# Attention and token mixer: the last 64 queries of two heads share one score tile

## What is computed

```
q_rot, k_rot = rotate(q), rotate(k)                    # rotary embedding
scores = (q_rot @ k_rot.T) / sqrt(64)                  # 576 x 576 for each head
attn   = exp(scores - max(scores)); attn /= sum(attn) + 1e-9
x      = heads side by side of attn @ v                # [4, 576, 512]
h      = relu(x.T @ w_tok1) @ w_tok2                   # mixing over positions
u      = x + h.T
out    = u + relu(u @ w_ch1) @ w_ch2                   # mixing over channels
```

## Time and profile before

| | before |
|---|---|
| median of 3 runs (lowest to highest) | 741.0 us (741.0 to 745.12) |
| the profiled execution | 744.22 us, of which the span (first to last instruction) is 742.5 |
| TensorE matmul (PE) busy | 698.0 us, 94% of the span |
| VectorE (DVE) / ScalarE (ACT) / GpSimd (POOL) busy | 401.4 / 344.8 / 229.7 us |
| granted TensorE clock, mean | 0.995 |

### The profile page before, as it was taken

How to read it: one execution, slowest core, us unless ns; L and a number is a source line. 1 busy time by engine, 2 the same in 40 slices (tenths; PEclk the granted TensorE clock), 3 DMA queues, 4 the chain that set the end, 5 groups by cost and what they waited for, 6 DMA issues and landing times.

```text
span 742.5 us, 13143 instructions
## 1 busy us (share of the span) xinstructions
PE 698.0 (94%) x5104; PEld 657.6 (89%) x5104; DVE 401.4 (54%) x644; ACT 344.8 (46%) x743; POOL 229.7 (31%) x257
## 2 busy tenths in 40 slices
PE   2799999999999999988899999999999999999996
PEld 1688888898888888887799998999989999899996
DVE  6588998888888988887661213212232122221211
ACT  3488888888888888876340203102022021220110
POOL 3967777777777777222000000000000000000000
PEclk9999999999999999999899999999999999999999
DMA  8655666655666555760520001200012000000000
GB/s 225 151 143 147 153 159 147 152 149 145 156 141 149 148 147 124 180 233 17 187 72 1 29 1 36 72 1 29 1 36 71 0 28 0 12 25 1 29 1 35
DMA packets 58421, 65.56 MB, mean 88 GB/s; under 512 B 18432, under 2 KB 42112, under 8 KB 58368
## 3 DMA queue, kind: packets, MB, share of 16 engines
q1 hardware_dynamic: 58368, 64.84, 32.7%
HBM read 29.16 MB, written 9.44 MB: 52 GB/s over the span
## 4 chain that ended last, share of the span: by engine, by line
PE 50%; DVE 1%; ACT 1%; issue 0%; ACTq 0%
PE slot L903 14%; PE slot L904 14%; PE slot L902 14%; PE slot L943 4%; PE slot L936 1%; PE slot L990 1%; PE slot L166 1%; PE slot L169 1%; ACT x_hi L149 1%; PE slot L168 0%; DVE x_lo L154 0%; DVE x_hi L158 0%; ACTq L867 0%; DVE out_t L1111 0%; DVE out_t L1114 0%
## 5 line engine op out<-in xcount | busy, mean ns | idle before, releaser
L629 ACT ACTIVATE prob<-slot,neg_max 128x576 f32<-128x576 f32 x160 | 117.5, 737 | 41.4 <-DVE neg_max L719 41.4
L719 DVE TENSOR_REDUCE neg_max<-slot 128x1 f32<-128x576 f32 x160 | 115.2, 752 | 38.9 <-PE slot L503 38.0
L1036 ACT ACTIVATE h_hi<-slot 128x512 fp32r<-128x512 f32 (+1 forms) x48 | 31.3, 652 | 184.2 <-PE slot L904 184.2
L902 PE MATMUL slot<-ut_hi,w_ch_hi 128*128 128x320 f32 (+1 forms) x384 | 114.0, 297 | 0.0
L904 PE MATMUL slot<-ut_hi,w_ch_lo 128*128 128x320 f32 (+1 forms) x384 | 113.7, 296 | 0.0
L903 PE MATMUL slot<-ut_lo,w_ch_hi 128*128 128x320 f32 (+1 forms) x384 | 113.7, 296 | 0.0
L902 PE MATMUL slot<-h_hi,w_ch_hi 128*128 128x320 f32 (+1 forms) x384 | 113.7, 296 | 0.0
L903 PE MATMUL slot<-h_lo,w_ch_hi 128*128 128x320 f32 (+1 forms) x384 | 113.7, 296 | 0.0
L904 PE MATMUL slot<-h_hi,w_ch_lo 128*128 128x320 f32 (+1 forms) x384 | 113.7, 296 | 0.0
L1081 DVE SCALAR_TENSOR_TENSOR h_lo<-slot,h_hi 128x512 fp32r<-128x512 f32 (+1 forms) x56 | 41.5, 748 | 119.6 <-ACT h_hi L1036 112.9
L559 PE MATMUL slot<-ident,prob 128*128 128x128 f32 (+1 forms) x640 | 87.4, 276 | 1.8
(11 more groups left out here) (88 smaller groups left out, 1317.4 us busy)
## 6 DMA issues: line engine op xcount, KB each, us to landing
q_hi<-t_hi_q SPq DMA_DIRECT2D x32, 160.0 KB, 2.5
q_cross<-t_lo_q SPq DMA_DIRECT2D x32, 160.0 KB, 2.6
q_cross<-t_hi_q SPq DMA_DIRECT2D x32, 160.0 KB, 2.7
key<-t_hi_k SPq DMA_DIRECT2D x32, 160.0 KB, 2.8
key<-t_lo_k SPq DMA_DIRECT2D x32, 160.0 KB, 2.9
raw_qk<-in_q_dram SPq DMA_DIRECT2D x16, 256.0 KB, 2.7
raw_qk<-in_k_dram SPq DMA_DIRECT2D x16, 256.0 KB, 2.6
raw_v<-in_v_dram SPq DMA_DIRECT2D x16, 256.0 KB, 2.7
```

What stands on the lines that cost most here:

```text
L629: act.activation(prob[a][:, t, 0:S].rearrange("p (f n) -> p f n", f=2), slot[(a * NG + t) % 2][:, :, 0:HALF], ACT.Exp, bias=neg_max[a][:, ...
L719: dve.tensor_reduce(neg_max[a][:, t:t + 1], slot[(a * NG + t) % 2][:, :, 0:HALF], AX.XY, ALU.max, negate=True).then_inc(maxed[t], 1)
L902: pe.matmul(ps, lhs[0], rhs[0], start=first, stop=False)
L1036: act.activation(h2[0][:, 2 * i:2 * i + 2, 0:n], unit_slot(k)[:, :, 0:n], ACT.Relu).then_inc(hi_done, 1)
```

## The change

Heads are worked on in pairs, an even head and the odd one after it. The pair's last 64 queries share one tile: the raw q of the tail is laid block-diagonally (head 0's tail in partitions 0 to 63 and channel half 0, head 1's in partitions 64 to 127 and half 1, zeros elsewhere), so that column group 4 of the transposed q holds 64 queries of each head, and the tile's 128 rows are scored in three passes straight from `t_hi` and `t_lo` of q and k (six matmuls instead of four). The even head has five score tiles, the odd one four: nine for a pair. The same holds for `maximum`, `exponent`, the sums and the reciprocals (one for a pair).

The shared tile is transposed once, in two units of the even head: unit 5 (four 128×128 transposes) for the first 512 keys and unit 6 (one transpose) for the last 64. Their columns go to both ends of `pt_hi` and `pt_lo`, which become 640 wide: head 0's tail queries in columns 0 to 63, head 1's in 576 to 639, the main ones between. The odd head has units 0 to 4 alone. Each of units 5 and 6 is one instruction on ScalarE and one on VectorE.

```diff
-    UNIT_BANK = (3, 0, 1, 2, 3, 2)
+    TILES_PAIR = 2 * G + 1
+    UNIT_BANK = ({6: 2, 0: 3, 5: 2, 1: 0, 2: 1, 3: 2, 4: 3}, {0: 3, 1: 2, 2: 0, 3: 1, 4: 3})
+    UNITS = ((6, 0, 5, 1, 2, 3, 4), (0, 1, 2, 3, 4))
...
+                if t < G:
+                    cols = slice(t * P, (t + 1) * P)
+                    passes = ((q_hi[a][:, cols], key[a]), (q_cross[a][:, cols], key[a]))
+                else:
+                    pe.wait_ge(t_lo_done, 2 * p + 2)
+                    cols, i = slice(MAIN, W), p % 2
+                    passes = ((t_hi["q"][i][:, cols], t_hi["k"][i]), (t_hi["q"][i][:, cols], t_lo["k"][i]),
+                              (t_lo["q"][i][:, cols], t_hi["k"][i]))
...
-                    pe.wait_ge(pt_lo_done[1], m - 3)
-                    pe.wait_ge(pt_lo_done[2], m - 3)
+                    pe.wait_ge(pt_lo_done, units_until(m - 4, 2 if m % 2 == 0 else 3))
...
                 act.wait_ge(pt_ready, units_until(h, u))
+                if u == UNITS[a][0] and h > 0:
                     act.wait_ge(pv_ready, h)
...
+                elif u == 5:
+                    part, ps = tail_columns(pt_hi[:, 0:G, :]), ps.rearrange("p (j e n) -> p j e n", j=G, e=2)
                 else:
...
+                    part = tail_columns(pt_hi[0:TAIL, G:NG, :])
+                    ps = ps[0:TAIL, HALF:HALF + P].rearrange("p (j e n) -> p j e n", j=1, e=2)
+                act.activation(part, ps, ACT.Copy).then_inc(pt_hi_done, 1)
...
+                copy_o(odd - 2)
+                p_hi(even, 6)
+                exponent(odd, 2)
...
+                p_lo(even, 6)
+                maximum(odd, 2)
+                output(odd - 2)
```

More of the change, by code:

```diff
@@ L370, in step @@
                     assemble_k(0, buf)
-                late = isinstance(s, int) and s < 2
-                if ahead and not late:
+                if ahead and s >= 2:
                     sp.wait_ge(products, s * 2 + 10)
@@ L384, in step @@
                         assemble_k(1, buf)
-                if ahead and late:
+                if ahead and s < 2:
                     sp.wait_ge(products, s * 2 + 10)
                     load("qk"[a], p + 3)
[L389 to L395, removed]
+            for s in range(N):
+                step(s)
             for c in range(CT):
@@ L437, in normalise @@
                 if no(h):
                     return
[L439 to L445, removed]
-            for m in (2, 3):
-                rotate(pool, "qk"[m % 2], m)
@@ new lines, in values @@
+                a = h % 2
+                pe.wait_ge(v_split, h + 1)
+                for f in range(2):
+                    at = a * D + f * HALF
+                    for j in range(NG):
+                        if f == 0 and j in (0, G):
+                            pe.wait_ge(pt_lo_done, units_until(h, 3 if j == 0 else 4))
+                        for pt in ((pt_hi, pt_lo) if j < G else (pt_hi,)):
+                            mm = pe.matmul(V_SLOT[:, f, 0:HALF], v_sb[a][:, j, :], pt[:, j, at:at + HALF],
+                                           start=(j == 0 and pt is pt_hi), stop=(j == NG - 1))
@@ new lines, in turn_p @@
+                mm.then_inc(pt_ready, 1)
+            transpose_qk(0)
+            transpose_qk(1)
+            for p in range(N // 2):
+                even, odd = 2 * p, 2 * p + 1
+                score(even, 0)
+                if p < N // 2 - 1:
+                    transpose_qk(even + 2)
+                score(even, 1)
+                values(even - 2)
+                score(even, 2)
+                score(even, 3)
+                transpose_o(even - 2)
+                turn_p(even - 1, 0)
+                turn_p(even - 1, 1)
+                score(even, 4)
+                turn_p(even - 1, 2)
+                turn_p(even - 1, 3)
+                turn_p(even - 1, 4)
+                score(odd, 0)
+                if p < N // 2 - 1:
+                    transpose_qk(odd + 2)
+                score(odd, 1)
+                turn_p(even, 6)
+                values(odd - 2)
+                score(odd, 2)
+                transpose_o(odd - 2)
+                turn_p(even, 0)
+                turn_p(even, 5)
+                score(odd, 3)
+                for u in range(1, NG):
+                    turn_p(even, u)
```

531 lines of the change are left out of this document (256 added, 275 removed).

## The result

| | before | after |
|---|---|---|
| median (lowest to highest), 4 runs each | 741.07 us (741.0 to 745.12) | 748.19 us (747.77 to 748.53) |
| profiled execution (span) | 744.22 (742.5) | 748.53 (746.7) |
| busy PE / DVE / ACT | 698.0 / 401.4 / 344.8 | 677.7 / 383.8 / 326.7 |
| a pair in attention | 19.73 | 20.18 |
| the mixer's first transposes start at | 356.46 | 361.76 |

What follows compares the result with a forecast made beforehand. Attention's loop of waits through VectorE, TensorE and ScalarE bounds the kernel. A pair goes from 19.74 to 20.43, +10.4 over 15 pairs, +8.6 with the ends: median 741.0 to 749.6 us, range 738 to 757.

Steps and rivals of the forecast that it cites:

- lower bound of 0.4: Odd step, VectorE: least delay of maximum 2 behind unit 6, if both pieces of unit 6 take next to nothing.
- M to T: Start of maximum 2 on VectorE to start of the q/k transposes on TensorE: 5.44 in both steps, 5.53 before.
- T to S: Start of the q/k transposes to start of score tile 1, both on TensorE: 0.59 in both steps, as before.
- S to the end of v: Odd step, TensorE: start of score tile 1 to the end of the product with v, 3.24 instead of 3.02.
- end of v to M: Odd step: end of the product with v to maximum 2, queued behind unit 6's rest: 1.38, 0.65 later than before.
- S to M: Start of score tile 1 to the next maximum 2: 3.75 as before into the even step, 4.62 into the odd.
- the floor of 2.15 after M: Odd step: unit 0's rest starts 2.15 after maximum 2, needing ScalarE's exponential 2 and unit 0; removed cover gains nothing.
- the switch of "Work removed": TensorE: one more switch from transposes to matmuls a pair, costing 0.11 on top of unit 6's own 0.11.
- The two paths "without a gap": From maximum 2 to score tile 1 in before, through VectorE and through ScalarE: both 6.12, ScalarE's without a gap.
- B: Rival, chance 0.15: the wait is hidden because VectorE gets unit 6 before score 2 is read; pair 19.78, 740 us.
- C: Rival, chance 0.12: TensorE's sum of work paces attention's loop, so each pair saves 0.49; 732 us.
- D: Rival, chance 0.07: TensorE loses its clock in attention's odd-step gaps, a slow step costing up to 9; 759 to 768.

Runs made afterwards that it cites:

- e1: The kernel after with maximum 2 of the odd head put ahead of the rest of unit 6 on VectorE: 738.33 us, ratio to before 0.9933.
- e2: The kernel after with the rest of unit 6 computed once more on VectorE, into a spare tile ahead of the real one: 751.95 us.
- b2: The kernel before without VectorE's 64x64 rest of unit 5 (zeros in its place): 737.87 us.
- e3: The kernel after with only the last of the five output transposes of each head on TensorE: 747.48 us.
- e6: e1 with score 3 and its maximum early, exponential 3 between units 2 and 3 in the odd step; the like in the even step, other banks: 737.96 us.

## Why the prediction was right, and where its sizes were off

**The cause was right.** The queue order on VectorE was to cost 0.65 a pair. From the end of v to the maximum it cost 1.35 - 0.73 = 0.62, and e1 and e2 show that it is this instruction. (The lower bound of 0.4 that the prediction gave for this delay is no bound: with both pieces of unit 6 at nothing its own sum is 0.20 + 0.57 + 0.03 + 0.02 - 0.73 = 0.09.) The rest of unit 6 writes partitions 64 to 127 and the maximum behind it all of them, and it starts only at 175.18, behind the end of the rest (174.87 + 0.28); the two rests of e2, both in the upper half, start 0.21 apart at a length of 0.28. The Trainium skill (VectorE: DVE Perf Modes, Two Vector instructions with no wait between them) has the rule: an instruction whose output starts in another quarter of the partitions than the last one's is held until all earlier ones have finished. The trace agrees: held for the 0.28 and 0.03 more, against 0.21.

**Leg by leg, forecast and measured.**

| leg of a pair | forecast | measured |
|---|---|---|
| even M to T | 5.44 | 5.44 (164.78 to 170.22) |
| T to S | 0.59 | 0.49 (to 170.71) |
| S to the end of v | 3.24 | 3.12 (to 173.83) |
| end of v to M | 1.38 | 1.35 (to 175.18) |
| odd M to T | 5.44 | 5.44 (to 180.62) |
| T to S | 0.59 | 0.58 (to 181.20) |
| S to M | 3.75 | 3.76 (to 184.96) |
| sum | 20.43 | 20.18 |

The order within both M-to-T legs came out as worked: unit 3 in the place of unit 5, the floor of 2.15 after M, and TensorE's idle 0.83 ahead of the odd step's unit 3.

**The terms that were too large: "T to S is 0.59" and the switch of "Work removed".** Three terms carry the 0.25 between the two sums.

- The 0.59 was read in the earlier trace rows as the time from the transposes to score 1 and kept for both new steps. What it measured was the ScalarE path that ended 0.05 before S. With that path early, as in the new even step, five transposes take 0.49. The text itself said that both paths tie, so the figure had two owners and the prediction gave it to one. In the new odd step ScalarE binds again, and 0.58 is back.
- "One more switch costs 0.11" was counted on top of 0.11 for unit 6. In the trace unit 6 starts at 171.33 and the second v matmul comes at 171.57. S to the end of v grew from 3.02 to 3.12 in all, so the transpose and its switch together are 0.10.
- The handover behind `copy_o` was 0.03 shorter.

**The two paths "without a gap" of before** were a misreading too (b2): the row x3 hid a wait. It changed no forecast number, because the chain through unit 5's bank ends at the same S. It does mean that before's loop hung on a 64x64 instruction, worth 0.20 of each step's 9.87.

**The ends.** By the mixer's start, attention took 5.3 longer and not 8.6. The start was 0.28 earlier (forecast 0.5), the 14 pairs up to the last added 0.43 each on average, or 6.0 (forecast 14 × 0.69, or 9.7), the last pair 0.14 from its even to its odd maximum 2 (forecast 0.69 - 0.2), and the tail gave back 0.59 (forecast 1.1: the idle 1.09 of the earlier trace rows is gone, but VectorE idles 0.98 for ScalarE at 350.02 now).

**The median** came 1.4 below the forecast: the terms above took 3.3 off (8.6 to 5.3), and 1.8 came back, which lies within the spread of the clock at the mixer's start. That the median came so near is in part luck: attention's share was forecast 3.3 too high. The 3.2 by which the profiled execution of before lay over its median is about the 3.4 us that the clock took there; the prediction carried it along without knowing its place.

**The rivals.** B fell: maximum 2 did not get ahead. C fell by e3. D did not come in the attention of after: its windows stand at 1.00 up to 362 us in spite of gaps of 0.87. The risk was real all the same: the clock did fall near the end of attention in e1, e3 and e6, once each and at a cost of 1.5 us, where D had priced a slow step at up to 9. And the two matmuls of the earlier trace rows that took 0.69 look like the low level: in e3 two of this size take 0.68 while the clock is low (343.73) and 0.42 at the full one. The trace of before has no record of the clock ahead of 36.0 us, so the 1.00 that its view shows there is no measurement.

## What to carry to other kernels

A wait is paid not only by the instruction that needs it, but by everything behind it in that engine's queue: when a small new piece is put into an order, ask what it waits for, and put the instruction that others wait for ahead of it. Removing work from engines that wait for each other in a loop gives only what lies on the loop, and a duration read between two marks belongs to whichever of the paths ended last. A merged row of a timeline can hide a wait: compare its length with the sum of single steps before calling a path gapless. And before a difference below one per cent is explained, look at the granted clock of each trace over the whole span, not only at the place that is compared.

## What the runs showed of the hardware

- The granted clock fell to 0.5, that is to 1.2 GHz, where attention ends and the mixer begins, after TensorE had been busy 1.55 of 4 us in before and 1.91 of 4 in after. It stood there for 6.8 us in before and 3.4 in after. e3 kept the full clock at this place after the same 1.91 of 4, but had lost it for 3.4 us at 342.6, after TensorE had been busy 0.63 of 2 us; after, with 0.65 of 2 us at the same place, did not. So how busy TensorE was just before doesn't settle it; what does is open.
- What the low clock costs: the same 18 matmuls with v take 2.46 us from the first start to the next product at the full clock and 3.99 where the clock is low for most of them (e1, e3 and e6).
- One transpose (128x128) set between matmuls of 288 columns costs 0.10 with all switching; five in a row, with TensorE idle before them, take 0.49 until the next matmul starts (170.22 to 170.71 in after).
- A 64-partition VectorE instruction that writes the upper half holds the next one, which writes all partitions, until its end (0.28 + 0.03 from start to start); behind one that writes the upper half too it does not (0.21, in e2).
